# Zero matmuls, one-pass products, one transpose, tensor-tensor norms and later stores in a delta-rule attention followed by two feed-forward layers

## The reference

```python
def _attn_ref(q, k, v, beta):            # B=4, H=8, S=768, D=48
    k_n = k / (norm(k) + 1e-6)
    state = zeros(B, H, D, D)
    for t in range(S):
        y[t] = q[t] @ state
        v_old = state.T @ k_n[t]
        state = state + beta[t] * outer(k_n[t], v[t] - v_old)
def _moe_ref(x, w_in, w_out, a, b):      # 3072 tokens, 384 -> 2048 -> 384
    h = x @ w_in
    g = (a0 + a1*h + a2*h^2 + a3*h^3) / (1 + |b0||h| + |b1|h^2 + 1e-6)
    return g @ w_out
def _moe2_ref(x, w_in, w_out):
    return relu(x @ w_in)**2 @ w_out
# out = _moe2(_moe(_attn(...)))
```

## Time and profile before

| | us |
|---|---|
| median of 3 runs | 1175.11 |
| lowest, highest | 1173.97, 1175.12 |
| the profiled execution | 1175.11 |
| its span | 1173.4 |
| PE busy, share of the span | 1105.7, 94% |
| DVE, ACT, POOL busy | 724.0, 655.0, 435.5 |

### The profile page before, as it was taken

The page is one execution under the profiler, slowest core; times in us unless marked ns, Lnnn a source line. Parts: engine busy times, 40 slices in busy tenths (PEclk is TensorE's granted clock), DMA queues, the critical chain, the costliest instruction groups (busy, mean ns, idle before and its releaser), DMA issues.

```text
span 1173.4 us, 18180 instructions
## 1 busy us (share of the span) xinstructions
PE 1105.7 (94%) x6352; PEld 964.7 (82%) x6352; DVE 724.0 (62%) x1239; ACT 655.0 (56%) x1311; POOL 435.5 (37%) x499
## 2 busy tenths in 40 slices
PE   4858888999998899999999999999999999999998
PEld 4858888999997678888888888778888888888886
DVE  5946696584335998878788887876333333333332
ACT  3455555754446977777787877755242333333332
POOL 4047018108302987777787777810000000000000
PEclk9968898999999999999999999999999999999999
DMA  5762765854444201010010103033010101010000
GB/s 124 147 137 61 172 137 125 176 98 100 102 129 120 83 1 54 1 38 17 1 54 1 54 1 108 1 109 107 1 54 1 54 1 54 1 50 5 1 28 27
DMA packets 173626, 74.41 MB, mean 63 GB/s; under 512 B 135968, under 2 KB 161696, under 8 KB 172576
## 3 DMA queue, kind: packets, MB, share of 16 engines
q1 hardware_dynamic: 173536, 73.26, 25.4%
HBM read 52.27 MB, written 20.71 MB: 62 GB/s over the span
## 4 chain that ended last, share of the span: by engine, by line
PE 63%; DVE 3%; ACT 1%; issue 1%; ACTq 0%; DVEq 0%
PE ps_y L1099 11%; PE ps_y L1100 11%; PE ps_y L1101 11%; PE ps_h L1084 10%; PE ps_h L1085 10%; PE ps_h L1086 10%; DVE ps_h L1255 1%; DVE w_in_lo L1218 1%; DVE cubic L1233 0%; DVE ps_h L1239 0%; DVE w_out_lo L1221 0%; DVE g_hi L1248 0%; DVE g_lo L1263 0%; ACT w_in_hi L1122 0%; ACT coef L1142 0%
## 5 line engine op out<-in xcount | busy, mean ns | idle before, releaser
L1084 PE MATMUL ps_h<-x_hi,w_in_lo 128*128 128x512 f32 x576 | 226.9, 394 | 14.4 <-DVE g_lo L1263 7.6
L1085 PE MATMUL ps_h<-x_lo,w_in_hi 128*128 128x512 f32 x576 | 226.1, 393 | 0.0
L1086 PE MATMUL ps_h<-x_hi,w_in_hi 128*128 128x512 f32 x576 | 226.0, 392 | 0.0
L1099 PE MATMUL ps_y<-g_hi,w_out_lo 128*128 128x512 f32 x576 | 224.5, 390 | 0.1
L1101 PE MATMUL ps_y<-g_hi,w_out_hi 128*128 128x512 f32 x576 | 224.4, 390 | 0.0
L1100 PE MATMUL ps_y<-g_lo,w_out_hi 128*128 128x512 f32 x576 | 224.4, 390 | 0.0
L1274 DVE TENSOR_TENSOR q<-h_sq 128x512 f32<-128x512 f32 x96 | 66.4, 691 | 135.3 <-ACT h_sq L1163 133.8
L1084 PEld LDWEIGHTS ps_h<-x_hi,w_in_lo 128*128 128x128 f32 x576 | 109.4, 190 | 39.2 <-DVE g_lo L1263 9.3
L1170 ACT ACTIVATE g_hi<-q 128x512 fp32r<-128x512 f32 x96 | 60.7, 633 | 141.7 <-PE ps_y L1101 137.2
L1343 POOL TENSOR_TENSOR head_times_q<-q,g_hi 128x512 f32<-128x512 f32 x96 | 124.4, 1296 | 10.8 <-DVE g_hi L1248 10.8
L1086 PEld LDWEIGHTS ps_h<-x_hi,w_in_hi 128*128 128x128 f32 x576 | 109.2, 190 | 22.8
(11 more groups left out here) (103 smaller groups left out, 1982.4 us busy)
## 6 DMA issues: line engine op xcount, KB each, us to landing
kq<-kq_in SPq DMA_DIRECT2D x10, 768.0 KB, 6.4
shared<-w_in SPq DMA_DIRECT2D x32, 192.0 KB, 4.1
shared<-w_out SPq DMA_DIRECT2D x32, 192.0 KB, 4.3
vkp<-k_in SPq DMA_DIRECT2D x12, 384.0 KB, 5.5
vkp<-v_in SPq DMA_DIRECT2D x12, 384.0 KB, 5.6
iq<-kq_in SPq DMA_DIRECT2D x12, 384.0 KB, 4.3
x_first<-y_t SPq DMA_DIRECT2D x24, 192.0 KB, 2.4
shared<-x_first SPq DMA_DIRECT2D x6, 768.0 KB, 5.9
```

Source lines behind the costliest of these rows:

```text
L1084: pe.matmul(bank(n), lo, x_hi[:, slot, k, :], start=(k == 0), stop=False)
L1085: pe.matmul(bank(n), hi, x_lo[:, slot, k, :], start=False, stop=False)
L1086: mm = pe.matmul(bank(n), hi, x_hi[:, slot, k, :], start=False, stop=(k == KT - 1))
L1099: pe.matmul(ps_y[m][:, :], lo, g_hi[:, d, :], start=(f == 0), stop=False)
```

## The change

- TensorE runs `warm(14)` before its first products, and `warm(20)` after the products of group 15, once ScalarE has copied group 8's P: matmuls of zeros (128x128 by 128x384) into bank 0, of which nothing is read before other results are written there. `neg_cross` is set to zero first for it.
- The first eight groups use `products` as well: keys and queries in one matmul with 128 columns, where there were two with 64. `k_diag` has two slots for all groups, so that `spread_keys(j)` waits for the products of `j-2`.
- `take_first_n` of these groups is three operations of 64 rows by 128 elements, which put the blocks of both halves into the same columns, so that `turn_blocks` is one transpose of 128 rows.
- The four quads' norms are one chunk. In `scales`, the two TENSOR_SCALAR operations become a TENSOR_TENSOR and a SCALAR_TENSOR_TENSOR with a tile of two constants (`limits`).
- `scale_v` goes to GpSimd but for quads 1 and 2, and so does the mask of P of groups 8 to 15; ScalarE places two parts of quad 0 rather than three, VectorE two, by TENSOR_TENSOR max rather than a copy. GpSimd starts round 1 once VectorE's parts are placed.
- VectorE's `take_products` stands ahead of the inversion's pieces in a step. Round 2 is spread over the steps up to 15, where it was 14, and its inverse is stored at step 15.
- SyncE's first loads have another order; `load_kq(3)` is ahead of `move_cross`, `load_kq(4)` ahead of `load_q(1)` and `load_v(1)`. `store_y` is one step later.

```diff
-    INV_TO = (None, 6, 14, 21, 29, 37)
-    NORM_CHUNKS = ((0, 1), (2, 3)) + tuple((h,) for h in range(4, QUADS))
+    INV_TO = (None, 6, 15, 21, 29, 37)
+    V_BY_DVE = (1, 2)
+    WARM_FIRST, WARM_LATER = 14, 20
+    NORM_CHUNKS = ((0, 1, 2, 3),) + tuple((h,) for h in range(4, QUADS))
...
-                if n >= 3 and n % 2 == 1:
-                    store_y((n - 3) // 2)
+                if n >= 4 and n % 2 == 0:
+                    store_y((n - 4) // 2)
...
+            scale_v(0)
+            pool.wait_ge(placed_by_dve, 2)
+            invert(1, 0, INV_OPS)
+            for g in range(FIRST, UPFRONT):
+                mask_products(g)
+            for h in (3, 4, 5):
+                scale_v(h)
+            invert(3, 0, INV_OPS)
+            for h in (6, 7, 8, 9):
+                scale_v(h)
+            invert(5, 0, INV_OPS)
+            for h in (10, 11):
+                scale_v(h)
...
+            def warm(count):
+                zeros = neg_cross[:, :, :].rearrange("r p d -> r (p d)")
+                for _ in range(count):
+                    pe.matmul(banks[0][:, 0:PAIRS * D2], zeros[:, 0:P], zeros, start=True, stop=True)
...
+            pe.wait_ge(const_ready, ZERO_CONST)
+            warm(WARM_FIRST)
+            for g in range(UPFRONT):
                 products(g)
+            pe.wait_ge(p_copied, FIRST + 1)
+            warm(WARM_LATER)
...
-                dve.tensor_scalar(work[0], root[:, mine], 1e-18, None, ALU.max).then_inc(norm_step, 1)
+                dve.tensor_tensor(work[0], root[:, mine], limits[:, 0:1].to_broadcast([P, cols]),
+                                  ALU.max).then_inc(norm_step, 1)
...
+                if g < FIRST:
+                    dve.tensor_tensor(mine[later, :, 0:BL], np_bank(g)[later, :, 0:BL],
+                                      by[later].to_broadcast(shape), ALU.mult)
+                    dve.tensor_tensor(mine[earlier, :, 0:BL], np_bank(g)[earlier, :, BL:C],
+                                      by[earlier].to_broadcast(shape), ALU.mult)
+                    dve.tensor_tensor(mine[earlier, :, BL:C], np_bank(g)[earlier, :, 0:BL],
+                                      by[earlier].to_broadcast(shape), ALU.mult).then_inc(n_first, 1)
...
+                dve.transpose(inv[:, 0].rearrange("q j i -> q i j"),
+                              n_all[:, :, :, 0:BL].rearrange("j a q i -> j i (a q)")).then_inc(blocks_turned, 1)
...
             for n in range(LAST_MM):
+                if n > 0 and end_group(n - 1) is not None:
+                    take_products(end_group(n - 1))
                 for r in INV_FROM:
...
-                if n > 0 and end_group(n - 1) is not None:
-                    take_products(end_group(n - 1))
```

More of the change, by code:

```diff
@@ L314, in _ @@
             sp.dma_start(beta[:, :], beta_in).then_inc(beta_loaded, 16)
[L315 to L321, removed]
+            for h in range(1, 4):
+                load_k(h)
+            for h in range(2):
+                load_first_k(h)
+                load_first_q(h)
             load_v(0)
@@ L658, in _ @@
             act.preload_act_table_set("sqrt_and_others")
-            squares(0)
-            squares(1)
+            for h in range(4):
+                squares(h)
+            act.wait_ge(const_ready, HALF_CONST)
             roots(0)
-            act.wait_ge(const_ready, HALF_CONST)
-            spread_keys(0)
-            squares(2)
-            spread_keys(1)
-            squares(3)
-            roots(1)
-            spread_keys(2)
-            spread_keys(3)
+            for j in range(4):
+                spread_keys(j)
             for g in range(FIRST):
@@ L734, in scales @@
                 dve.wait_ge(norm_step, step + 4)
-                dve.tensor_scalar(norm[:, mine], work[3], 0.5, 1e-6, ALU.mult, ALU.add).then_inc(norm_step, 1)
+                dve.scalar_tensor_tensor(out=norm[:, mine], in0=work[3], scalar=0.5,
+                                         in1=limits[:, 1:2].to_broadcast([P, cols]), op0=ALU.mult,
+                                         op1=ALU.add).then_inc(norm_step, 1)
                 dve.wait_ge(norm_step, step + 5)
@@ L832, in turn_inverse, with place_quad @@
                               ).then_inc(inverse_turned, 1)
+            def place_quad(quad, s):
+                dst, src = place(quad, s)
+                dve.tensor_tensor(dst, src, src, ALU.max).then_inc(placed_by_dve, 1)
             def mask_products(g):
@@ L842, in inverted @@
                 return INV_OPS * (n - INV_FROM[r]) // (INV_TO[r] - INV_FROM[r])
-            sums(0)
-            sums(1)
+            for h in range(4):
+                sums(h)
             dve.wait_ge(beta_loaded, 16)
@@ L848, in _ @@
             scales(0)
-            sums(2)
-            for g in range(4):
-                take_first_n(g)
-            sums(3)
-            scales(1)
-            for g in range(4, FIRST):
+            for g in range(FIRST):
                 take_first_n(g)
@@ L860, in _ @@
             dve.wait_ge(const_ready, CONSTS)
-            scale_v(0)
             dve.wait_ge(inverse_turned, 1)
-            dve.tensor_copy(*place(0, 3)).then_inc(placed_by_dve, 1)
+            for s in range(2, SUB):
+                place_quad(0, s)
             sums(4)
             for n in range(LAST_MM):
+                if n > 0 and end_group(n - 1) is not None:
+                    take_products(end_group(n - 1))
                 for r in INV_FROM:
```

146 lines of the change are left out of this document (72 added, 74 removed).

## The result

| us | before | after |
|---|---|---|
| median of 4 runs, run in turn on one chip | 1174.88 | 1161.81 |
| lowest, highest | 1173.97, 1175.12 | 1160.17, 1163.34 |
| the profiled execution | 1175.11 | 1163.14 |
| its span | 1173.4 | 1161.4 |

The ratio is 0.989, with a 95% interval of 0.9871 to 0.9908. The interval lies clear of 1, so the change is faster, by about 1.1%. The gain is 13.1 us where 17.3 were forecast, and 1161.81 lies inside the range.

A forecast was written before the change was run, and what follows sets the result against it. TensorE's own work bounds the loop from z(16) on, so only z(16)'s start can move. 13.3 + 5.0 + 8.3 - 9.3 = 17.3 us gained, from 1175.1 to 1157.8 us, range 1146 to 1167.

The forecast's parts named there:

- What bounds it: Attention loop from z(16) on: TensorE's own work, 5.79 us a step; the change can only move z(16)'s start, 198.45 us.
- Before the loop: Stage up to the first start_z: loop starts at 55 rather than 68.32 us, 13.3 us gained (bounds 52 and 59).
- The last term: End of the stage before the loop: warm(20) ends at 55 us, behind the parts placed at 51.9, and sets the start.
- Steps 0 to 8: From start_z(0) to z(8): 2.3 us gained up to z(0), 5.0 in both stretches (bounds 1 and 10).
- the slow clock of the first step: Early attention loop: the slow clock ahead of the 3.43 us wait goes, about 2.7 us.
- Step 8's wait stays: TensorE's wait for the inverse at step 8 remains, its store being issued behind loads that fill the DMA queue.
- Steps 8 to 15: Attention loop, z(8) to z(16) in the prediction: take_products first and work off VectorE, 8.3 us gained (bounds 4 and 9.8).
- Step 16: TensorE stands 7.6 us for round 2's inverse, stored at step 15, then a slow clock: 9.3 us lost (bounds 0 and 11).
- (a): Rival at step 16: no stall, as the store or its DMAs overtake or 8.75 us is too much; 1148.5 us, chance 0.22.
- (c): Rival before the loop: zeros do not raise the clock at all, loop starts at 71.6; 1179.4 us, chance 0.04.
- (b): Rival before the loop: clock falls between warm(14) and the products or in their gaps, start at 61; 1163.8 us, chance 0.10.

The follow-up runs named there:

- the run that removes the stall: Changed kernel with INV_TO[2] back at 14, so round 2's inverse is stored in step 14: 1151.51 us, ratio 0.9805.

## Why the prediction was right, point by point

**What bounds it.** Right: z(16) slid by 11.96 us and the span by 12.0; a step from 16 on is 5.79 us.

**Before the loop, 13.3 forecast, 13.9 measured.** Every link held within about a microsecond. The maximum took 0.23 us (0.25 forecast) at 12.85; the scales were ready at 16.0 (16.3); the products began at 13.99 (14.4) and took 7.41 us; the scaling of N cost 0.83 us a group (0.7) and ended at 22.7 (22.9); the blocks were turned at 24.9 (25.0); `take_n(8)` began at 27.57 (28); the parts were placed at 52.04 (51.9); the zeros ended and the loop started at 54.45 (55). The last term hides a slip: the prediction's own 28 + 11.2 + 1.5, then 12.8 and 2.3 to 3 more, make 55.8 to 56.5 and not 55. Nor is 54.45 a typical start. With the same code it came at up to 57.38, so the gain of this stage is 10.9 to 13.9 us by the profile that one takes. No run put back the one-pass products or the single transpose, so their shares are read from the rows and not shown by a run. The exclusive lock named from the Trainium skill, "SBUF — State Buffer", section "SBUF: two separate sides" (one instruction holds the shared ports, and a VectorE operation with two SBUF inputs is not held up by a GpSimd operation that reads nothing), agrees with both forms here, 2.72 and 0.23 us under one memset. What the prediction did not say is that little of a gain in this stage may reach the end: without the first zeros, or with the old norms, the loop starts 3.5 and 3.6 us later, the attention's end moves by -0.5 and +0.6 in the one profile of each, and the median by +0.1 and +2.0.

**Steps 0 to 8: the mis-sized term.** Forecast were 2.3 (measured 2.3) and 2.7 more, of which came -1.3. The part named for it, the slow clock of the first step, came with 1.7: z(0) to z(1) took 6.11 us after 7.81. It was given back in the next two. z(1) to z(2) took 12.89 after 12.17, and z(2) to z(3) 10.32 after 8.45. The prediction had put the two-input placing at "0.1 to 0.3 us dearer a piece, the norms a little cheaper". The placing was 0.3 dearer a piece (2.11 against 1.49 for two), the norms of step 1 were no cheaper, 3.3 us against 3.2, and the wait rose from 3.43 to 4.19. That was within what I had read, but I costed it at nothing, and not what can follow from it: the wait of step 3 rose from 1.14 to 1.73 and has a low clock behind it here. The run with copies took back some 0.5 us a wait. The low clock is a matter of the execution: the same program had the full one in step 3 with the store at step 14. So is much of the whole miss. z(0) to z(8) took 63.6, 66.8, 67.0 and 67.1 us in the four other profiles whose code is the same up to step 6, a gain of 0.6 to 4.1 where this one shows a loss of 1.3; the 63.6 had the full clock in steps 3 and 8. The kernel before scatters as well: with its order changed from step 7 on it took 66.8 us rather than 67.6. What is shown beyond the scatter is the half microsecond a wait by which the two-input placing was under-priced; that the other 3 to 3.5 us of the miss are more than chance is not shown. "Step 8's wait stays" was right (3.04 us).

**Steps 8 to 15.** 8.3 forecast, 9.2 measured, and its cause held: 4.1 to 4.4 from the order, 4.3 from the work taken off VectorE, the rest with the eighth step of the inversion.

**Step 16: right in kind, too small.** The forecast was a wait of 7.6 us and its slow clock, 9.3 in all, from a round trip of 8.75 us. The round trip was 11.7 us (167.69 to 179.38), the wait 10.0, the loss 12.2. I had taken the trip from step 8, where the store has the key load ahead but not six more DMAs of `store_n(8)`. I did see those, but counted only SyncE's time for them, 3.6 us (3.57 measured). Nor is the trip of step 8 a constant: in the changed kernel it took 10.3 us (108.75 to 119.09), and in the seven others with the same list 9.9 to 10.3, against 11.3 to 11.7 at step 16. The run with the store first shows that SyncE's time is nearly worthless: with it removed, TensorE began 0.5 us sooner. What was mis-sized is the time from the store's start to the landing of the load; which of the transfers around it makes it longer stays open.

**The rivals.** (a), no stall at step 16, did not happen; its price, 9.3, is 12.2 from z(15) to z(16) and 10.3 in the time, by the run that removes the stall. (c) falls with one row: 28 records of zeros in 11.60 us, where 0.64 us each would make 17.9, and products at 0.93 us a group behind them. Zeros raised the clock here. (b) did not happen in this profile, but it was no idle worry: in four of the eleven profiles with these zeros the clock did fall in the gap behind them, and the products took 9.04 us. That these gaps were 1.70 us or more, and here 1.13, is luck as far as the prediction goes. So is a part of the total: the low clocks of steps 3 and 8 went against the forecast, the early start with it.

## What to carry to other kernels

Do not price a moved DMA by the moment at which the engine that issues it gets there. Here a store to be read back through DRAM needed a whole step more than the trip measured elsewhere would have had it, and issuing it 2.9 us sooner gave 0.5. And a wait costs what follows it: here a tenth of a microsecond more or less went with 1.5 us of low clock, and it went both ways for the same program. So a gain ahead of such waits should be followed to the end of the stage, and in more than one execution, before it or its loss is put down to an edit.

## What the runs showed of the hardware

- A one-input VectorE operation of 128x64 elements stood until GpSimd's memset was over (2.72 us); the two-input form took 0.23 us under the same memset. Placing two pieces of 32x512 elements took 0.87 us as a copy and 1.40 as a two-input maximum with GpSimd idle, and 1.49 to 1.58 and 2.04 to 2.11 beside GpSimd's two-input inversion: both forms took 0.6 to 0.7 us more there, and the copy is the cheaper one either way.
- The same four DMAs of the inverse took 1.90 us to start in one run and 5.40 in another, where ten other DMAs had been started in the 5.7 us before.
- Matmuls of zeros brought TensorE to the full clock, and an idle time of 1.70 to 2.01 us behind them was followed by a clock of 0.50 in four of four profiles, one of 0.72 to 1.19 us in none of seven.
- The same program, run again, had the low clock behind a wait of 1.6 us or not, which is worth 1.5 us. z(7) to z(8) took 7.8 to 11.6 us behind waits of 1.9 to 3.1 us for the inverse, by whether the low clock came.
- The second block, the same instructions each time, took 802.6 to 806.8 us in fourteen profiled executions.
